# Gate products inside attention, and slots inverted to tokens so that experts gather rows of x

## The chip, the cores and the metric

The kernel runs on one core of a Trainium2 chip. The metric is the device time in microseconds of one launch, which covers all stages. Inputs and output are float32 arrays in HBM.

## What is computed

```python
# attention: B, H, S, D = 4, 8, 768, 40; for every step t of S
y[:, :, t] = einsum('bhd,bhde->bhe', rt, state)
Sa = einsum('bhde,bhe->bhd', state, at)
state = state * wt - outer(Sa, bt) + outer(vt, kt)
x = y.transpose(0, 2, 1, 3).reshape(3072, 320)
# routed experts: E = 8, F = 1024
noisy = x @ w_gate + log1p(exp(x @ w_noise)) * noise
top2, top2_w = the two largest of the 8 and their softmax
out[token] = sum over its two experts e of top2_w * (relu(x[token] @ w1[e]) @ w2[e])
# feed-forward: h = out @ w_in (320 x 2048), g = h * tanh(softplus(h)), result g @ w_out
```

## The kernel before

`build` runs four stages one after another: `attention`, `route`, `experts`, `mish_ffn`. Each is a `Block` in which every engine has its own instruction list; at its end all engines meet at a barrier.

**attention** works on 8 groups of 4 heads (GR = 8), 12 chunks of 64 steps each. One TensorE list is written out by the string `ORDER`: single letters `u`, `s`, `r` are the hops of the recurrence, short and each waiting for the one before; the tokens with a digit (`N0`, `K1`, `F0`, `X1`) are wide steps of 6 to 48 matmuls into one of three PSUM buffers `wide`, which are placed between the hops. ScalarE (`BY_ACT`) or VectorE takes each buffer away. `Y` makes the output transposed in `yT`; `X` (L431 to L436) turns `yT` back into rows of tokens, six transposes a step, and ScalarE copies them to `xr` (L511 to L516). There are 16 X steps, two per group. SP stores `xr` to `x_by_pair` in HBM. Near the start ScalarE's queue also writes zeros to all of `slots` (L522).

**route** reads x back (L719) into `xg`, tokens on partitions, 24 tiles of 128. TensorE transposes each tile (L758), ScalarE and VectorE copy it (L774, L799), and TensorE multiplies it by the gate weights into `plog` (L746). Then VectorE makes the noisy logits, the two best experts, ranks within each expert (two matmuls, L766 and L767) and `pos`, the slot of each token's two choices (L803 to L852). Slots are sorted by expert, padded to 55 tiles of 128 (M = 55). GpSimd scatters the rows of `xg` to `slots` by 48 indirect DMAs (L739), each of which follows the last one, and waits until they have landed. `tile_expert` (L857) tells which expert each tile belongs to. SP loads the down weights of all experts after the noise (L721 and L1223).

**experts** runs over the 55 tiles: SP loads a tile of `slots` into `xs` (L903) and that expert's up weights (L909, L911), TensorE transposes x (L932), multiplies up (L943, L948) and down (L962). VectorE copies the result and GpSimd's queue stores it to `results` (L922). TensorE's list is hidden(t), turn_x(t+1), output(t-1).

**mish_ffn** gathers each token's two result rows by indirect DMAs on `pos` (L1073), mixes them and runs the feed-forward.

## Time and profile before

| what | us |
|---|---|
| median of 3 runs (lowest, highest) | 1735.26 (1734.24, 1742.23) |
| the profiled execution | 1734.15 |
| its span | 1732.4 |
| attention, until the barrier behind it | 595.4 |
| route, until the experts' first transfer | 138.2 |
| experts, until the last stage's first transfer | 539.5 |
| TensorE busy in the span | 1458.0 (84%) |
| VectorE, ScalarE, GpSimd busy | 582.3, 580.1, 285.8 |

The stage bounds are the first instructions behind each barrier at 595.40, 733.64 and 1273.17 us. A time of the profile counts from the start of the span. The granted clock of TensorE is 0.5 where it is at 1.2 GHz and 1.0 where it is at 2.4 GHz. Lines named L... are those of the kernel before.

### The profile page before, as it was taken

Reading aid. Unit: us, or ns where it says so; the run is one execution under the profiler, and the core shown is the slowest. Engines: PE = TensorE matmul, PEld = TensorE weight load, DVE = VectorE, ACT = ScalarE, POOL = GpSimd, SP = SyncE. Lnnn points to the kernel's source line nnn. Section 1 sums busy time; section 2 is a strip of 40 time slices with the busy share of each in tenths; the row PEclk is TensorE's granted clock in tenths of the full one; section 3 lists DMA queues with packets and bytes.
Section 4 is the critical chain, followed back from the end, with each engine's and each line's share of the span. In section 5 each row is a group of like instructions: output and inputs, shape, how many; then the busy total and the mean of one; then the engine's idle time right before and its main releaser. Section 6 shows DMA issues by size and latency. Waiting matters only on the chain. (4 is left out here: it accounts for less than half of the span.)

```text
span 1732.4 us, 42914 instructions
## 1 busy us (share of the span) xinstructions
PE 1458.0 (84%) x18753; PEld 1126.9 (65%) x18753; DVE 582.3 (34%) x1120; ACT 580.1 (33%) x1145; POOL 285.8 (16%) x253
## 2 busy tenths in 40 slices
PE   1687887888897590089999999999948999999999
PEld 1577776777786490078888888888823555555556
DVE  8454664564543113000000000000016545445441
ACT  0353554454453110011121211212108454555541
POOL 5333223223210004600000000000041101000000
PEclk9878998888887655589999999999969999999999
DMA  7524134224111292375656555565361101000000
GB/s 213 154 52 111 45 76 117 66 54 117 47 46 42 56 298 76 111 241 162 186 163 184 174 169 186 159 188 166 105 185 35 31 23 31 27 23 12 8 12 19
DMA packets 127671, 180.66 MB, mean 104 GB/s; under 512 B 68384, under 2 KB 96800, under 8 KB 126208
## 3 DMA queue, kind: packets, MB, share of 16 engines
q1 hardware_dynamic: 113184, 144.16, 29.1%
q0 software_dynamic: 7248, 24.75, 4.3%
q10 hardware_dynamic: 7056, 9.01, 1.5%
q8 instruction: 151, 2.47, 0.6%
q14 instruction: 32, 0.26, 0.1%
HBM read 144.13 MB, written 33.75 MB: 103 GB/s over the span
## 5 line engine op out<-in xcount | busy, mean ns | idle before, releaser
L962 PE MATMUL pY<-down,hT 128*128 x880 | 245.9, 433 | 0.0
L998 DVE COPY ys<-pY 128x320 f32<-128x320 f32 x55 | 27.0, 491 | 570.9 <-PE pY L962 570.9
L943 PEld LDWEIGHTS pH<-exT,up 128*128 128x128 f32 x1760 | 207.7, 194 | 14.5 <-DMA up_rest<-in_moe_w 4.4
L943 PE MATMUL pH<-exT,up 128*128 128x128 f32 x1760 | 208.3, 277 | 5.4 <-DMA up_rest<-in_moe_w 3.9
L1108 PE MATMUL mpY<-wout,h 128*128 128x320 f32 x768 | 210.4, 433 | 0.0
L962 PEld LDWEIGHTS pY<-down,hT 128*128 128x128 f32 x880 | 163.0, 190 | 61.2
L989 ACT ACTIVATE hT<-pH 128x512 f32<-128x512 f32 x110 | 59.7, 594 | 422.1 <-PE pH L948 422.1
L1108 PEld LDWEIGHTS mpY<-wout,h 128*128 128x128 f32 x768 | 144.3, 190 | 60.7 <-issue 3.0
L1095 PE MATMUL mpH<-mxT,win 128*128 128x512 f32 x384 | 173.2, 605 | 4.9 <-ACT mxT L1137 4.7
L1095 PEld LDWEIGHTS mpH<-mxT,win 128*128 128x128 f32 x384 | 74.0, 194 | 92.1 <-issue 82.7
L1145 ACT ACTIVATE act_in<-act_in 128x512 f32<-128x512 f32 x96 | 59.9, 629 | 183.2 <-DVE act_in L1184 183.2
L922 POOL DMA_DIRECT2D results<-ys x55 | 29.8, 541 | 509.5 <-DVE ys L998 509.5
L1175 DVE TENSOR_TENSOR h<-h,act_in 128x512 f32<-128x512 f32 x96 | 59.9, 685 | 142.8 <-ACT act_in L1151 142.7
L932 PE MATMUL pX<-ident,xs 128*128 128x128 f32 x110 | 24.4, 304 | 75.4 <-DMA xs<-slots 75.4
L1184 DVE TENSOR_SCALAR act_in<-mpH 128x512 f32<-128x512 f32 x96 | 65.4, 682 | 59.4 <-PE mpH L1098 59.4
L1073 POOL DMA_INDIRECT rows<-results,pos x48 | 45.7, 953 | 230.8 <-DVE mix L1163 214.7
L484 ACT ACTIVATE npow<-wide 128x768 bf16<-128x768 f32 x80 | 63.3, 810 | 55.8 <-PE wide L373 37.9
L484 ACT ACTIVATE uv<-chain 64x80 f32<-64x80 f32 x192 | 44.1, 230 | 93.8 <-PE chain L456 92.3
L282 POOL TENSOR_TENSOR kbT<-kbT,after 128x1536 f32<-128x1536 f32 x16 | 55.0, 3457 | 107.6 <-DMA kbT<-in_kb 107.6
L411 PE MATMUL wide<-rblk,uvT 80*128 80x128 f32 x384 | 61.4, 324 | 6.7 <-issue 5.7
L1185 DVE COPY h<-mpH 128x512 f32<-128x512 f32 x96 | 65.1, 678 | 0.0
L932 PEld LDWEIGHTS pX<-ident,xs 128*128 128x128 f32 x110 | 11.2, 142 | 82.4 <-DMA xs<-slots 75.9
(168 smaller groups left out, 2167.7 us busy)
## 6 DMA issues: line engine op xcount, KB each, us to landing
up<-in_moe_w SPq DMA_DIRECT2D x55, 1024.0 KB, 5.3
up_rest<-in_moe_w SPq DMA_DIRECT2D x110, 128.0 KB, 5.3
down<-in_moe_w SPq DMA_DIRECT2D x8, 1280.0 KB, 14.7
slots<-zero_row ACTq DMA_DIRECT2D x1, 8800.0 KB, 36.2
xs<-slots SPq DMA_DIRECT2D x55, 160.0 KB, 5.2
results<-ys POOLq DMA_DIRECT2D x55, 160.0 KB, 2.2
wfr<-in_wdec SPq DMA_DIRECT2D x16, 480.0 KB
kbT<-in_kb SPq DMA_DIRECT2D x16, 480.0 KB
```

Source lines behind the costliest of these rows:

```text
L282: nc.gpsimd.tensor_tensor(kbT[:, i], kbT[:, i], backwards, ALU.mult).then_inc(kb_scaled, 1)
L411: m = pe.matmul(out[:, bank, place], uvT[half][:, i, c].rearrange("q s f -> q (s f)"), rblk[half][:, i, c].rearrange("q h f -> q (h f)"), ...
L484: return nc.scalar.activation(out, in_, ACT.Copy, scale=scale)
L943: pe.matmul(pH[t % 2][b][:, c, :], up[t % NU][:, k, f * P:(f + 1) * P], xT[t % 2][:, k, :], start=(c == 0 and k == 0), stop=False, skip_gr ...
L962: m = pe.matmul(pY[t % 2][:, 0:D], hT[t % 2][:, j, :], down[:, bass.ds(e, 1), j, :].rearrange("q n d -> q (n d)"), start=(j == 0), stop=(j ...
L989: nc.scalar.activation(hT[t % 2][:, b * HT:(b + 1) * HT, :], pH[t % 2][b][:], ACT.Relu).then_inc(h_copied[b], 1)
L1095: pe.matmul(pH[f % 4][:], win[:, k, f * P:(f + 1) * P], xT[g % 2][:, k, :], start=(k == 0), stop=False)
L1108: m = pe.matmul(pY[t % 2][:, 0:D], h[g % 2][:, f, j * P:(j + 1) * P], wout[:, f, :], start=(f == 0), stop=(f == FT - 1))
L1145: nc.scalar.activation(a[:, f, :], a[:, f, :], ACT.Exp).then_inc(exped, 1)
L1175: nc.vector.tensor_tensor(at, at, act_in[n % 3][:, f, :], ALU.mult).then_inc(gated, 1)
L1184: nc.vector.tensor_scalar(act_in[n % 3][:, f, :], pH[f][:], 20.0, None, ALU.min).then_inc(h_min, 1)
L1185: nc.vector.tensor_copy(h[g % 2][:, GT * q + f, :], pH[f][:]).then_inc(h_used, 1)
```

## The change

The routing stage no longer touches x. In attention the X step multiplies `yT`, which has the features on the partitions, by the gate weights of the group's heads (`gw`, loaded once) into 48 free columns of the same PSUM buffer. Two groups make up one batch element's features: the second one adds the sum so far, which is in `logits`, by a matmul with the identity. ScalarE copies the 48 columns to `logits`.

In `route`, after `pos` is known as a float, each slot is split into its tile (of 55) and its row (of 128). For each of the 48 pairs of token tile and choice, VectorE makes `row_hot` (a token's row as 0/1 over 128) and, over the 55 tiles, the token's tile number where it matches; GpSimd makes the same with the row of the token. TensorE multiplies and sums over all 48, so that `slot_token` holds for each slot the number of its token. In `experts`, GpSimd gathers the rows of x by indirect DMAs on `slot_token`. The scatter to `slots`, `slots` itself and its zeros are gone. The noise transfer is the first of its stage on SP's queue and the down weights follow.

```diff
+                    if g == 0:
+                        pe.wait_ge(gate_loaded, 16)
+                    else:
+                        taken(pe, tok, g - 1)
+                    first, odd = g // 2 * (S // P) + half * (W // P), g % 2 == 1
+                    if odd:
+                        pe.matmul(out[:, 0, W:W + W // P * 2 * E], ident[:], logits[:, first:first + W // P, :].rearrange("q c n -> q (c n)"),
+                                  start=True, stop=False, skip_group_check=True)
+                    for j in range(W // P):
+                        for i in range(2):
+                            m = pe.matmul(out[:, 0, W + j * 2 * E:W + (j + 1) * 2 * E], yT[:, i, cols(j, P)], gw[:, g % 2 * 2 + i, :],
+                                          start=(i == 0 and not odd), stop=(i == 1), skip_group_check=True)
...
+                        copy(xr[:, i, rows, :].rearrange("q c (h d) -> q c h d", d=D),
+                             t[:, i, 0:W].rearrange("q (c h d) -> q c h d", h=2, d=64)[:, :, :, 0:D])
+                    first = g // 2 * (S // P) + half * (W // P)
+                    m = copy(logits[:, first:first + W // P, :], t[:, 0, W:W + W // P * 2 * E].rearrange("q (c n) -> q c n", n=2 * E))
...
-            act.wait_ge(kb_loaded, 32)
-            act.dma_start(slots.rearrange("(m q) d -> q m d", q=P),
-                          zero_row[:].unsqueeze(1).to_broadcast([P, slots.shape[0] // P, slots.shape[1]])).then_inc(slots_cleared, 16)
...
-            for b in range(B):
-                for j in range(4):
-                    sp.dma_start(xg[:, b * NC:(b + 1) * NC, j * 80:(j + 1) * 80],
-                                 x_by_pair[4 * b + j].rearrange("(c q) d -> q c d", q=P)).then_inc(rows[b], 16)
-            sp.dma_start(nz[:], noise.rearrange("(t q) e -> q t e", q=P)).then_inc(wload, 16)
+            sp.dma_start(nz[:], noise.rearrange("(t q) e -> q t e", q=P)).then_inc(nload, 16)
...
-            pool.wait_ge(placed, 1)
-            for t in range(T):
-                for k in range(2):
-                    nc.gpsimd.indirect_dma_start(out=slots, out_offset=bass.IndirectOffsetOnAxis(ap=pos[:, 2 * t + k:2 * t + k + 1], axis=0),
-                                                 in_=xg[:, t, :], in_offset=None).then_inc(sent, 16)
-            pool.wait_ge(sent, 32 * T)
...
+            pool.wait_ge(split_up, 1)
+            for j in range(2 * T):
+                nc.gpsimd.tensor_scalar(tile_hot[:, j, 1, :], minus_m[:], minus_tile[:, j // 2, j % 2:j % 2 + 1], row_of[:],
+                                        ALU.is_equal, ALU.mult).then_inc(by_pool, 1)
...
+            for j in range(2 * T):
+                pe.wait_ge(by_dve, j + 1)
+                pe.wait_ge(by_pool, j + 1)
+                m = pe.matmul(pinv[:], row_hot[:, j, :], tile_hot[:, j], start=(j == 0), stop=(j == 2 * T - 1))
+            m.then_inc(inverted, 1)
...
+            then(vec.tensor_scalar(tile_i[:], posf[:], 1.0 / P, None, ALU.mult))
+            then(vec.tensor_copy(tile_f[:], tile_i[:]))
+            then(vec.scalar_tensor_tensor(row[:], tile_f[:], -float(P), posf[:], ALU.mult, ALU.add))
+            then(vec.scalar_tensor_tensor(minus_tile[:], row[:], 0.0, tile_f[:], ALU.is_lt, ALU.subtract))
+            vec.scalar_tensor_tensor(row[:], minus_tile[:], float(P), posf[:], ALU.mult, ALU.add).then_inc(split_up, 1)
+            dve.wait_ge(split_up, 1)
+            for j in range(2 * T):
+                vec.tensor_scalar(tile_hot[:, j, 0, :], minus_m[:], minus_tile[:, j // 2, j % 2:j % 2 + 1], float(j // 2), ALU.is_equal, ALU.mult)
+                vec.tensor_scalar(row_hot[:, j, :], iota_row[:], row[:, j // 2, j % 2:j % 2 + 1], None, ALU.is_equal).then_inc(by_dve, 1)
+            then(vec.tensor_copy(pos[:].rearrange("q (t k) -> q t k", k=2), posf[:]))
...
+            dve.wait_ge(inverted, 1)
+            then(vec.tensor_copy(texp[:], pinv[:, 1, :]))
+            then(vec.scalar_tensor_tensor(slot_token[:], pinv[:, 0, :], float(P), texp[:], ALU.mult, ALU.add))
...
-            def load_x(t):
-
-                wait(sp, x_turned, t - 2)
-                sp.dma_start(xs[t % 3][:], xv[t]).then_inc(loaded[t % 3], 16)
...
+            def gather_x(t):
+
+                wait(pool, x_turned, t - 2)
+                nc.gpsimd.indirect_dma_start(out=xs[t % 3][:], out_offset=None, in_=x,
+                                             in_offset=bass.IndirectOffsetOnAxis(ap=slot_token[:, t:t + 1], axis=0)).then_inc(loaded[t % 3], 16)
+
+            for t in range(3):
+                gather_x(t)
             for t in range(M):
+                if t + 3 < M:
+                    gather_x(t + 3)
```

TensorE's list around X0 in attention, of a second group (g = 1) before, and now. `wide` is the PSUM buffer; the rows ahead and behind are F0 and F1 and the chain's last hop.

```order
L387 MATMUL wide<-tpow,npow 64x64 x23
L435 MATMUL wide<-ident,yT 128x128 [waits wide_taken_by_dve]
L435 MATMUL wide<-ident,yT 128x128 x5
L387 MATMUL wide<-tpow,npow 64x64 [waits wide_taken_by_dve,wide_taken_by_act]
L387 MATMUL wide<-tpow,npow 64x64 x23
L456 MATMUL chain<-rhs,w 64x40 [waits rhs_ready]
```

```order
L389 MATMUL wide<-tpow,npow 64x64 x23
L437 MATMUL wide<-ident,yT 128x128 [waits wide_taken_by_dve]
L437 MATMUL wide<-ident,yT 128x128 x5
L445 MATMUL wide<-logits,ident 128x48 [waits wide_taken_by_act]
L449 MATMUL wide<-gw,yT 128x16 x6
L389 MATMUL wide<-tpow,npow 64x64 [waits wide_taken_by_dve,wide_taken_by_act]
L389 MATMUL wide<-tpow,npow 64x64 x23
L471 MATMUL chain<-rhs,w 64x40 [waits rhs_ready]
```

Seven matmuls now stand between the transposes and F1. The end of VectorE's list in the routing stage, from the sum that gives the slot as a float (`posf`), before and now (two of the 48 pairs are shown):

```order
L850 TENSOR_REDUCE posf<-chosen 128x24
L852 CAST pos<-posf 128x2x24 [waits gate_steps]
L854 TENSOR_TENSOR past<-iota_m,last 128x440
L856 TENSOR_REDUCE texp<-past 128x55 [waits gate_steps]
L857 TENSOR_SCALAR tile_expert<-texp 128x55 [waits gate_steps]
```

```order
L823 TENSOR_REDUCE posf<-chosen 128x24
L827 TENSOR_SCALAR tile_i<-posf 128x48 [waits gate_steps]
L828 CAST tile_f<-tile_i 128x48 [waits gate_steps]
L829 SCALAR_TENSOR_TENSOR row<-tile_f,posf 128x48 [waits gate_steps]
L830 SCALAR_TENSOR_TENSOR minus_tile<-row,tile_f 128x48 [waits gate_steps]
L831 SCALAR_TENSOR_TENSOR row<-minus_tile,posf 128x48 [waits gate_steps]
L834 TENSOR_SCALAR tile_hot<-minus_m,minus_tile 128x55 [waits slots_split]
L835 TENSOR_SCALAR row_hot<-iota_row,row 128x128
L834 TENSOR_SCALAR tile_hot<-minus_m,minus_tile 128x55
L835 TENSOR_SCALAR row_hot<-iota_row,row 128x128
```

`pos` and `tile_expert` now come behind the 48 pairs. GpSimd's queue from the end of the routing stage into the experts, before and now:

```order
L733 AFFINE_SELECT before<-before 128x128 [waits gate_constants]
L739 DMA slots<-xg,pos 7040x320 [waits slots_known]
L739 DMA slots<-xg,pos 7040x320 x47
L663 UNCONDITIONAL_BRANCH [waits rows_sent]
L918 UNCONDITIONAL_BRANCH [waits barrier_Pool_Activation_PE_DVE_SP_gather]
L922 DMA results<-ys 128x320 [waits y_copied] x55
```

```order
L740 TENSOR_SCALAR tile_hot<-minus_m,minus_tile,row_of 128x55 [waits slots_split,gate_constants]
L740 TENSOR_SCALAR tile_hot<-minus_m,minus_tile,row_of 128x55 x47
L673 UNCONDITIONAL_BRANCH
L897 UNCONDITIONAL_BRANCH [waits barrier_Pool_Activation_PE_DVE_SP_gather]
L902 DMA xs<-x,slot_token 128x320 x3
L902 DMA xs<-x,slot_token 128x320 [waits x_turned]
L911 DMA results<-ys 128x320 [waits y_copied]
L902 DMA xs<-x,slot_token 128x320 [waits x_turned]
L911 DMA results<-ys 128x320 [waits y_copied]
```

The 48 scatters are gone from the routing stage, and a gather stands ahead of each store but the last three in the experts' stage.

## Rows read from the trace of the kernel before

**Rows 1.** Stages, by stretch: length, busy of PE, PEld, DVE, ACT, POOL, clock, DMA.
```profile
607.00:649.00 42.00, 41.63 (x207) 41.10 (x205) 7.12 (x23) 5.82 (x22) 0.00 (x0) 0.50 1.03 303
667.00:733.00 66.00, 0.00 (x0) 0.00 (x0) 0.90 (x2) 0.00 (x0) 46.09 (x48) 0.50 0.33 119
751.00:1271.00 520.00, 514.33 (x3631) 431.28 (x3630) 27.01 (x55) 95.08 (x267) 29.75 (x55) 1.00 0.53 165
```
**Rows 2.** Timeline (start, duration, engine, instruction), around the barrier behind attention.
```profile
591.81 0.63 ACT L484 ACTIVATE xr<-wide 128x240 f32<-128x240 f32 x2 [7.79 <-PE wide L435]
595.40 0.14 POOL L727 IOTA iota_e<- 128x8 f32 x1 [97.54 <-POOLq L94]
```
**Rows 3.** Timeline, VectorE's routing chain.
```profile
648.67 0.36 DVE L803 TENSOR_SCALAR relz<-plog 128x192 f32<-128x192 f32 x1 [4.32 <-PE plog L746]
...
651.52 0.36 DVE L807 TENSOR_TENSOR relz<-relz,lnz 128x192 f32<-128x192 f32 x1 [2.10 <-ACT lnz L780]
...
666.17 0.19 DVE L852 CAST pos<-posf 128x48 int32<-128x48 f32 x1
```
**Rows 4.** Timeline, start of the experts.
```profile
733.64 0.34 SPq L903 DMA_DIRECT2D xs<-slots  x1
...
741.17 4.21 PE L943 MATMUL pH<-exT,up 128*128 128x128 f32 x18 [3.91 <-DMA up_rest<-in_moe_w]
```
**Rows 5.** DMA: noise (L721) from issue to landing, and the down weights' issues.
```profile
DMA to landing us min/median/max: 4.9/4.9/4.9
```
```profile
down<-in_moe_w SPq DMA_DIRECT2D x8, 1280.0 KB, 14.7
```
**Rows 6.** VectorE prices: two operations with a pointer scalar (min/median/max ns), and a cast's timeline.
```profile
L1159 DVE TENSOR_SCALAR mix<-rows,gates x24: 376/379/407, 1282.2 to 1611.1; 128x320 f32<-128x320 f32 x24
L1161 DVE SCALAR_TENSOR_TENSOR mix<-rows,gates,mix x24: 550/550/602, 1282.7 to 1611.5; 128x320 f32<-128x320 f32 x24
```
```profile
22.83 0.20 DVE L626 CAST identh<-ident 128x128 bf16<-128x128 f32 x1
22.94 0.18 DVE L630 COPY eye<-ident 64x64 f32<-64x64 f32 x1
```
**Rows 7.** Timeline, VectorE beside GpSimd.
```profile
31.81 2.69 POOL L287 MEMSET aT<- 128x1536 f32 x2
```
```profile
31.84 2.74 DVE L630 CAST eyeh<-ident 64x64 bf16<-64x64 f32 x1
```
```profile
667.56 0.38 DVE L857 TENSOR_SCALAR tile_expert<-texp 128x55 int32<-128x55 f32 x1
```
**Rows 8.** Timeline, GpSimd's own operations.
```profile
5.95 0.28 POOL L268 TENSOR_SCALAR_AFFINE_SELECT n<-n 128x128 f32<-128x128 f32 x1
...
22.99 1.80 POOL L275 TENSOR_TENSOR aT<-aT,dec 128x768 f32<-128x768 f32 x1 [2.17 <-DVE dec L597]
```
**Rows 9.** Timeline, TensorE prices: a wide f32 product, and weight loads in the experts.
```profile
659.36 0.98 PE L766 MATMUL pbef<-both,before 128*128 128x192 f32 x2 [10.73 <-DVE both L824]
```
```profile
760.02 3.81 PEld L943 LDWEIGHTS pH<-exT,up 128*128 128x128 f32 x32
```
**Rows 10.** Stretches ahead of the barriers behind the routing and behind attention, columns as in rows 1.
```profile
729.00:729.50 0.50, 0.00 (x0) 0.00 (x0) 0.00 (x0) 0.00 (x0) 0.00 (x0) 0.50 0.00 0
```
```profile
594.50:595.00 0.50, 0.00 (x0) 0.00 (x0) 0.00 (x0) 0.00 (x0) 0.00 (x0) 0.50 0.00 0
```
**Rows 11.** Indirect reads of rows (L1073) to landing; a result's store and tile 4's first transpose.
```profile
DMA to landing us min/median/max: 2.9/3.3/7.5
```
```profile
761.29 0.59 POOL L922 DMA_DIRECT2D results<-ys  x1 [33.89 <-DVE ys L998]
...
774.50 0.44 PE L932 MATMUL pX<-ident,xs 128*128 128x128 f32 x2
```
**Rows 12.** Steady attention, columns as in rows 1; TensorE's waits for the scaled keys: us, times, longest.
```profile
120.00:480.00 360.00, 301.51 (x9272) 268.14 (x9271) 202.51 (x363) 170.04 (x429) 103.88 (x54) 0.87 0.32 78
```
```profile
PE wide L336 <- POOL kbT L282: 7.7, 3, 5.1
```

More of the change, by code:

```diff
@@ L69, in attention @@
     HOPS = 3 * NC - 2
+    E = gate_w.shape[2] // 2
     def group_of(tok, it):
@@ L210, in store @@
                 rows = slice(half * (HC // 2), (half + 1) * (HC // 2))
+                first, pair = g // 2 * S + half * W, g % 2 * 2
                 for i in range(2):
-                    sp.dma_start(out_v[2 * g + i][:, rows, :], xr[:, i, rows, :]).then_inc(x_stored[half], 16)
+                    sp.dma_start(x[first:first + W, (pair + i) * DD:(pair + i + 1) * DD].rearrange("(c q) d -> q c d", q=P),
+                                 xr[:, i, rows, :]).then_inc(x_stored[half], 16)
             sp.wait_ge(w_pads, 1)
@@ L652, in _, with route @@
                         take(tok, g)
-def route(nc, x_by_pair, w_gate, w_noise, noise, slots, pos, gates, tile_expert, ident, load_down):
+def route(nc, logits, noise, pos, gates, tile_expert, slot_token, ident, load_down):
     N, E = noise.shape
-    D = w_gate.shape[0]
     T = N // P
-    B = x_by_pair.shape[0] // 4
-    NC = T // B
     M = tile_expert.shape[1]
@@ L752, in _ @@
-            for t in range(T):
-                if t % NC == 0:
-                    pe.wait_ge(rows[t // NC], 64)
-                wait(pe, copied[t % 2], t // 2 - 1)
-                for k, (k0, kn) in enumerate(KT):
-                    m = pe.transpose(pT[t % 4][0:kn, k, :], xg[:, t, k0:k0 + kn], ident[:])
-                m.then_inc(turned, 1)
-                if t > 2:
-                    logit(pe, t - 3)
-            for t in range(T - 3, T):
-                logit(pe, t)
             pe.wait_ge(const, 2)
@@ L769, in _ @@
+            m.then_inc(inverted, 1)
         @block.scalar
         def _(act):
-            for t in range(0, T, 2):
-                act.wait_ge(turned, t + 1)
-                wait(act, logits, t - 3)
-                nc.scalar.activation(xT[t % 4][:, 0, :], pT[t % 4][:, 0, :], ACT.Copy)
-                nc.scalar.activation(xT[t % 4][0:96, 1:3, :], pT[t % 4][0:96, 1:3, :], ACT.Copy).then_inc(copied[0], 1)
             act.wait_ge(soft, 1)
```

113 lines of the change are left out of this document (47 added, 66 removed).

## Prediction

> **What bounds the kernel now.** I read the stage table first. In the expert stage TensorE works 514.33 of 520 us and in 607 to 649 us 41.63 of 42, but from 667 to 733 us neither TensorE, VectorE nor ScalarE does anything and only GpSimd works [rows 1]. So four stages run one after another (attention, routing, experts, feed-forward), each shut off by a barrier, and what a stage costs is its own longest path. The routing stage is where the change acts. Its path starts with the barrier after attention, 595.40 us [rows 2]. The rows of x are read back, and then TensorE is the path until the last gate product; VectorE starts at 648.67 [rows 3]. That stretch is 53.3 us. VectorE then ranks the tokens until it writes pos at 666.17: 17.5 us [rows 3]. GpSimd issues 48 scatters one by one; the next stage's first transfer is issued at 733.64 and its first matmul starts at 741.17 [rows 4]. From 595.40 to 741.17 is 145.8 us, of which the change keeps little.
>
> **Removed in routing.** All 72 transposes, 144 gate matmuls, their copies, the 16 reads of x and the 48 scatters go. VectorE can start at the barrier: minus 53.3 us. The scatters and what follows them, 666.17 to 733.64, go too: minus 67.5 us; what stands in their place is costed below. The 9 MB of zeros that were written to slots during attention's first microseconds go as well. I count nothing for them, since no wait in the sum is on that queue.
>
> **The VectorE chain that stays** is 17.5 us. In it the noise is used at 651.52, which is 2.85 us after the chain's start [rows 3]. The noise transfer is now the first thing of its stage and landed 4.9 us after its issue [rows 5], so VectorE waits about 2.3 us for it (0 if it lands within 2.85 us, 5 if the down weights queued right behind on SP's queue slow it). Five small operations on 128x48 that split a slot into tile and row follow; at the 0.19 us of the pos cast [rows 3] and a semaphore wait each, 0.24 us, that is 1.2 us.
>
> **The inversion** is new: for each of 48 columns VectorE makes one 128x55 and one 128x128 comparison in bf16, GpSimd one 128x55, TensorE one matmul. The nearest VectorE row is a comparison's sister with a pointer scalar: 379 ns for 320 elements [rows 6]. Its two-tensor neighbour of the same length takes 550 ns [rows 6]: 171 ns more for 320 elements, 0.53 ns each, which I read as the one-source form costing 0.53 ns an element. So 128 elements cost 379 - 192 x 0.53 = 0.28 us and 55 cost 0.24 us. The next instruction starts about 0.09 us before the former ends (22.83 plus 0.20 against 22.94 [rows 6]). So a pair costs 0.19 + 0.15 = 0.34 us and 48 pairs 16.3 us. If the pointer cost nothing it would be some 10 us.
>
> GpSimd works at the same time and takes part in that price. In this trace a 64x64 cast that started at 31.84 lasted 2.74 us, until the two memsets of GpSimd were done, and a 128x55 operation lasted 0.38 us, ending when a GpSimd descriptor instruction ended [rows 7]. So short VectorE operations with one source in SBUF stand still while GpSimd holds something. A GpSimd select over 128 elements lasts 0.28 us [rows 8]; for 55 elements I take 0.2. If each of the 48 blocks VectorE for its whole length, the inversion is 48 x (0.34 + 0.2) = 26 us; if only the data parts exclude one another it adds about half, 21 us. I take 21, since the fixed part of a short instruction is most of it, and keep 10 and 26.
>
> The Trainium skill, "SBUF — State Buffer", section "Who interferes with whom", says that a VectorE instruction in a 2-port mode and a GpSimd instruction take a shared port pair for the whole instruction, whichever comes first, and the other fully blocks. By that rule the inversion would be the 26 us and the time 1657. The 2.74 us row agrees with it; no row shows two short instructions alternating.
>
> TensorE's matmul per column is hidden: a 128x192 f32 product, two records, took 0.98 us at the low clock [rows 9]; 110 bf16 columns in one record cost at most a third of that, 0.33 us, less than a pair. After the last column VectorE does pos, past, texp and tile_expert, as before from 666.17 to 667.94, 1.77 us [rows 3, 7], and two more short ones: 2.3 us.
>
> Sum from the barrier: 17.5 + 2.3 + 1.2 + 21 + 2.3 = 44.3 us.
>
> **The next barrier.** Before, the DMA engines were idle from 729.0 on, yet the experts' first transfer came at 733.64, 4.6 us later; after attention they were idle from 594.5 and GpSimd began at 595.40, 0.9 us later [rows 2, 4, 10]. The difference is that GpSimd had transfers outstanding in one case. In the changed routing stage it has none, so I take 0.4 us (bounds 0.2 and 4.6).
>
> **First rows of the experts.** The first expert matmul came 7.5 us after the stage's first transfer, because of the up weights [rows 4]. SP is now free of the x loads, so the weights come a little earlier, but x is fetched by GpSimd with an indirect read: one issue of 1.0 us, a landing of 2.9 to 7.5 us by the like reads of the last stage [rows 11], then transposes and copies. I take 8.0 us, bounds 7.2 and 10.5. The down weights are the stage's next transfers, 8 of 1280 KB [rows 5], 10.5 MB; at the 303 GB/s of [rows 1] they take 35 us and are in at 632, before anyone asks.
>
> First expert matmul: 595.4 + 44.3 + 0.4 + 8.0 = 648.1 instead of 741.2, **minus 93.1 us**.
>
> **Steady experts.** POOL now holds a gather ahead of each store. The gather of tile t+3 stands behind the store of tile t-1, which waits for VectorE's copy. For t = 1 that store is issued at 761.29 and tile 4 is turned at 774.50 [rows 11]: 13.2 us less 0.6 and 1.0 for the issues and a landing of 3.3 (7.5 at worst) leaves 8 us (4). The gather is hidden and the stage keeps its length. If that cover were gone, each microsecond would count 55 times.
>
> **Added in attention.** Each of 16 X steps gets six matmuls with 128x128 f32 weights, and every second group one matmul of the identity over 48 columns. Such matmuls are bound by their weights: 32 loads in 3.81 us, 0.119 each [rows 9]. That is 16 x 6 x 0.119 = 11.4 us, and 8 more for the four odd groups, 1.0 us: 12.4 us of TensorE. From 120 to 480 us TensorE works 301.5 of 360 us [rows 12], in program order with the chain's short hops between, so I count most of it. What can hide it: TensorE waited three times, 7.7 us in all, for GpSimd's scaled keys behind X0 [rows 12], which does not move with X0; that takes 2.4 us off. I take 10 us on the path, bounds 4 and 15 (the extra may delay the hops, and ScalarE's third copy in X, below the 0.32 us of one of its two [rows 2], sits ahead of a hop's copy). At the end of attention that copy adds 0.2 us.
>
> **Total**: 1734.15 (the profiled execution; the span is 1732.4, 1.75 less) - 93.1 + 10.2 = 1651.3. The median of the three runs is 1.1 us above the profiled one, so I say 1652.
>
> **Rivals.**
> - *GpSimd sets the inversion*: a comparison with two pointers and two operations takes 0.5 us there instead of 0.2 and is excluded with VectorE's: 48 x 0.84 = 40 us, 1671. For it: GpSimd's two-input products cost 1.80 us for 768 elements, more than twice a VectorE element [rows 8]. Against: 55 elements at that rate are 0.13 us.
> - *Everything overlaps*: X hidden down to 4 us and no port trouble, 16.3 or 10 us: 1652 - 6 - 5 to -11 = 1635 to 1641. For it: one sixth of TensorE's time in attention is idle. Against: the only wait in it that I can name beside X is the 7.7 us taken off already.
> - *Attention pays twice*: the X step delays a hop as well as the wide steps behind it, 24 us instead of 10: 1666. For it: hops wait for each other in one chain. Against: TensorE works 301.5 of 360 us there, which leaves the hops little to hold up [rows 12].
> - *Slower than before*: the gathers gate the experts, since GpSimd takes its queue in order behind the store's wait. It needs landings of 8 us more than I took, plus 83/55 = 1.5 us per tile to eat the gain, about 13 us each; from there the time is above 1735. The worst like landing was 7.5 us [rows 11].
> - *The change does not shorten the stage as it says*: the down weights, now issued at once, become its end. At half the rate of [rows 1] they would land at 667 and the experts' weights behind them: 1679.
>
> **How the numbers follow.** Forecast (1640 to 1662) 64%, GpSimd-bound 11%, all overlapped 11%, attention twice 8%, down weights 3%, gathers slower than before 2%, near no change by several at once 1%. The range 1634 to 1672 takes in the first four and the unknowns' bounds, and leaves 6 to 15%. A measurement of this kernel tells 0.5% (8.7 us) from nothing; faster by more 0.97, within 0.01, slower 0.02.
>
> **What would show it.** VectorE's first routing operation right at the barrier; a wait of some 2 us before the noise is used; 48 pairs of comparisons spaced 0.34 (no contention) to 0.54 us (full exclusion); under 1 us from the last VectorE operation to the experts' first transfer; L943's first matmul some 8 us behind; expert tiles still 9.45 us apart; attention's end near 605 instead of 595. I would be wrong if a comparison costs over 0.5 us on either engine, or if the hops slip by more than TensorE's extra work.

## The result

The kernel after takes 1693.7 us (median of 4 runs, 1681.85 to 1701.33) against 1735.67 us before, a ratio of 0.974 with a 95% interval of 0.969 to 0.980. It is faster by 2.6%. The prediction said 1652 us, 1634 to 1672: the direction was right, the size was not, and the time lies 22 us above the range.

The profiled execution took 1690.76 us (span 1689.0), where the sum of the prediction was 1651.3. These 39.5 us can be placed stage by stage, as each stage is shut off from the next by a barrier:

| piece of the path | predicted | measured | error |
|---|---|---|---|
| attention's end, later than before by | 10.2 | 37.9 (595.40 to 633.31) | +27.7 |
| barrier to the first comparison | 21.0 | 19.35 (to 652.66) | -1.65 |
| inversion | 21 | 30.9 (to 683.58) | +9.9 |
| what follows the inversion | 2.3 | 0.5 (to 684.05) | -1.8 |
| barrier to the experts | 0.4 | 1.25 (to 685.30) | +0.85 |
| first fetch to first expert matmul | 8.0 | 8.05 (to 693.35) | 0 |
| first expert matmul to last copy, change | 0 | 523.1 instead of 524.2 | -1.1 |
| last copy of the experts to the next stage, change | 0 | 12.3 instead of 7.8 | +4.5 |
| feed-forward, change | 0 | 460.2 instead of 459.2 | +1.0 |

Two terms carry the error: attention and the inversion. A third, the barrier behind the experts, wasn't in the sum at all. What follows the inversion took 0.5 us and not 2.3, since VectorE made `pos`, `past`, `texp` and `tile_expert` by 671.5 us, while GpSimd was still at its comparisons.

### The profile page after: what moved, and what is told of

It is laid out like the page before. It is cut to its first block and busy times, and to the rows that moved or that the text cites. A ratio compares the mean times of both kernels' runs of the same rounds, so it can differ in the third digit from the quotient of the medians.

```text
span 1689.0 us, 43070 instructions
## 1 busy us (share of the span) xinstructions
PE 1474.6 (87%) x18793; PEld 1138.5 (67%) x18793; DVE 597.6 (35%) x1198; ACT 575.3 (34%) x1137; POOL 326.6 (19%) x311
## 5 line engine op out<-in xcount | busy, mean ns | idle before, releaser
L413 PE MATMUL wide<-rblk,uvT 80*128 80x128 f32 x384 | 72.2, 365 | 1.0 <-ACT uvT L499 1.0
L413 PEld LDWEIGHTS wide<-rblk,uvT 80*128 80x128 f32 x384 | 66.6, 270 | 2.5 <-ACT uvT L499 1.2
L338 PE MATMUL wide<-kbT,aT 40*64 40x64 f32 x768 | 23.4, 291 | 50.9 <-DVE mask_un L648 38.6
L471 PE MATMUL chain<-rhs,w 64*64 64x40 f32 x768 | 48.4, 247 | 20.1 <-issue 7.6
```

The lines of the kernel that those rows point to most:

```text
L413: m = pe.matmul(out[:, bank, place], uvT[half][:, i, c].rearrange("q s f -> q (s f)"), rblk[half][:, i, c].rearrange("q h f -> q (h f)"), ...
```

## The profile after

**Attention.** The timeline of the kernel after, around attention's end, answers to [rows 2] (start, duration, engine, instruction, and in brackets the idle time before it and what ended it):

```profile
612.09 0.63 ACT L499 ACTIVATE xr<-wide 128x240 f32<-128x240 f32 x2 [7.19 <-PE wide L449]
...
629.23 0.63 ACT L499 ACTIVATE xr<-wide 128x240 f32<-128x240 f32 x2 [13.41 <-PE wide L449]
629.75 0.22 ACT L499 ACTIVATE logits<-wide 128x48 f32<-128x48 f32 x1
```
```profile
633.31 0.14 POOL L726 IOTA iota_e<- 128x8 f32 x1 [109.82 <-POOLq L95]
```

The last X step and the barrier behind it come 37.9 us later than in [rows 2]. Next, the X step's own price: one step's gate products on TensorE's timeline, first at the full clock, then near the end, where the granted clock is 1.00 up to 611 us and 0.50 from 612 on, and the groups of matmuls by line and shape (busy us, mean ns of one, idle before):

```profile
138.91 1.41 PE L449 MATMUL wide<-gw,yT 128*128 128x16 f32 x12
```
```profile
610.23 1.82 PE L449 MATMUL wide<-gw,yT 128*128 128x16 f32 x12
```
```profile
L449 PE MATMUL wide<-gw,yT 128*128 128x16 f32 x192 | 25.1, 270 | 0.0
L437 PE MATMUL wide<-ident,yT 128*128 128x128 f32 x96 | 16.0, 310 | 4.8 <-DVE yT L593 4.3 <-ACT npow L499 0.2
L445 PE MATMUL wide<-logits,ident 128*128 128x48 f32 x16 | 2.7, 251 | 0.0
```

Six f32 matmuls leave twelve records, while the six transposes of a step leave six (96 for 16 steps). A step's products cost 12 x 0.117 = 1.41 us, not 0.71. (The records of a group overlap: one lasts 270 ns in the mean, yet 192 of them make 25.1 us.) All in all the new records are 25.1 + 2.7 = 27.8 us of busy time. The last view is attention as one stretch from its start to its end, of before and of after (length, busy of PE, PEld, DVE, ACT, POOL with counts, granted clock, DMA share, GB/s):

```profile
0.00:595.00 595.00, 451.95 (x13432) 400.11 (x13432) 319.89 (x548) 250.04 (x625) 162.93 (x96) 0.86 0.33 84
```
```profile
0.00:633.00 633.00, 500.74 (x13640) 450.82 (x13640) 324.20 (x547) 251.67 (x641) 163.37 (x96) 0.82 0.27 65
```

TensorE has 208 records more and is busy 48.8 us more. 27.8 of these are the new records; the other 21 are the same old instructions taking longer, and the granted clock fell from 0.86 to 0.82. Between 1.2 GHz (0.5) and 2.4 GHz (1.0), a mean clock c says that the engine was at the lower level for 2(1 - c) of the time: 167 us before, 228 us after (to some 6 us, since c has two digits).

**Routing.** The timeline of the inversion in the kernel after, first VectorE's comparisons, then GpSimd's (joined into one line of 48), TensorE's last products, and the experts' first fetch:

```profile
652.42 0.21 DVE L831 SCALAR_TENSOR_TENSOR row<-minus_tile,posf 128x48 f32<-128x48 f32 x1
652.66 0.25 DVE L834 TENSOR_SCALAR tile_hot<-minus_m,minus_tile 128x55 bf16<-128x55 f32 x1
652.83 0.28 DVE L835 TENSOR_SCALAR row_hot<-iota_row,row 128x128 bf16<-128x128 f32 x1
653.02 0.24 DVE L834 TENSOR_SCALAR tile_hot<-minus_m,minus_tile 128x55 bf16<-128x55 f32 x1
```
```profile
652.81 30.26 POOL L740 TENSOR_SCALAR tile_hot<-minus_m,minus_tile,row_of 128x55 bf16<-128x55 f32 x48 [17.77 <-DVE row L831]
685.30 1.19 POOL L902 DMA_INDIRECT xs<-x,slot_token  x1 [2.23 <-POOLq L673]
```
```profile
682.67 0.25 PE L752 MATMUL pinv<-tile_hot,row_hot 128*128 128x110 bf16 x1 [0.29 <-POOL tile_hot L740]
683.22 0.25 PE L752 MATMUL pinv<-tile_hot,row_hot 128*128 128x110 bf16 x1 [0.30 <-POOL tile_hot L740]
```

A pair of VectorE's comes every 0.36 us and the last ends at 669.87 us. GpSimd is then still at it for 13 us, and TensorE waits for it each time. The tile's own view (min/median/max ns) has the price of each:

```profile
L834 DVE TENSOR_SCALAR tile_hot<-minus_m,minus_tile x48: 237/242/310, 652.7 to 669.4; 128x55 bf16<-128x55 f32 x48
L740 POOL TENSOR_SCALAR tile_hot<-minus_m,minus_tile,row_of x48: 564/646/965, 652.8 to 682.5; 128x55 bf16<-128x55 f32 x48
```

**Experts.** The first expert matmul, the landings of the gathers, and the last copy with the next stage's first transfer, 12.3 us apart:

```profile
693.35 5.33 PE L932 MATMUL pH<-exT,up 128*128 128x128 f32 x32 [1.00 <-DMA up_rest<-in_moe_w]
```
```profile
DMA to landing us min/median/max: 2.9/2.9/6.8
```
```profile
1216.49 0.49 DVE L987 COPY ys<-pY 128x320 f32<-128x320 f32 x1 [3.81 <-PE pY L951]
```
```profile
1228.82 0.84 SPq L1042 DMA_DIRECT2D win<-in_moe_w_in  x2
```

The same two rows of the kernel before, 7.8 us apart:

```profile
1265.37 0.49 DVE L998 COPY ys<-pY 128x320 f32<-128x320 f32 x1 [3.81 <-PE pY L962]
```
```profile
1273.17 0.84 SPq L1053 DMA_DIRECT2D win<-in_moe_w_in  x2
```

## Experiments on attention: records or clock

Two questions stood open: is it the products at all, and if so, their own time or the clock that went with them? The runs in this section are compared by their times and by attention's end, read as the start of GpSimd's first instruction behind the barrier. An end is that of one execution, the profiled one. From it to the end of the span it took 1054.1 to 1057.4 us in the nine profiled executions whose later stages are those of the kernel after (the fused one adds a single VectorE addition), so the ends of the other executions can be estimated as their span less 1056: 624 to 644 for the kernel after, 589 to 612 without products, 603 to 612 with 128 columns.

The end moves with the clock even where the program is the same. The kernel after, its repetition, and the two runs below in which ScalarE makes the second comparison or issues the stores have the same attention with 13640 records in it. They ended it at 633.31, 633.35, 640.30 and 651.83 us, with TensorE busy for 500.7, 500.6, 509.2 and 517.4 us and a granted clock of 0.82, 0.81, 0.80 and 0.79. The last of them:

```profile
0.00:651.00 651.00, 517.43 (x13640) 464.69 (x13640) 324.51 (x547) 251.63 (x641) 163.95 (x96) 0.79 0.27 63
```

**Without the products.** In the X step all six gate matmuls, the addition of the former group and the copy of the logits go, so that the noise alone routes:

```
-                        for j ...: for i ...: m = pe.matmul(out[:, 0, W + ...], yT[:, i, ...], gw[...], ...)
-                    m = copy(logits[:, first:first + W // P, :], ...)
+                            m = pe.transpose(out[:, i, cols(j, P)], yT[:, i, cols(j, P)], ident[:])
```

> Leaves out the gate products: attention makes no logits (they stay zero and the noise alone routes), everything else is the kernel after. Theory A (the 208 new matmul records are the cause, by their own time, 27.8 us, and by the lower granted clock that goes with them, some 21 us on the others, less idle time that closed): attention's last copy ends near 595 us, as before, against 633 after, the window of attention has TensorE busy 452 us at a clock of 0.86 instead of 501 us at 0.82, and the whole is 38 us shorter, 1652 us. Rival B (the attention of the kernel after is long for another reason, the transfers of gate weights, the wait for the logits' copy or a clock that happened to be low in that execution): the end stays above 615 us.

Measured: 1662.4 us (1646.6 to 1669.7), ratio 0.955 (0.947 to 0.963), attention's end at 605.29 us. The products, with the copy that goes with them, are the cause: 31 us come back. The end isn't at 595, though: this execution had a clock of 0.85 and so 182 us of low clock instead of 167.

**Half of them.**

```
-                        for i in range(2):
-                            m = pe.matmul(..., yT[:, i, cols(j, P)], gw[:, g % 2 * 2 + i, :], ...)
+                        m = pe.matmul(..., yT[:, 0, cols(j, P)], gw[:, g % 2 * 2, :], ...)
```

> Leaves out every second gate product (the upper half of each group's rows of the gate weights), 96 of the 192 product records; routing differs. Theory A with a cost in proportion to the records: attention's end half way, near 614 us, time 1672 us. Rival C (the cost comes in a step, because the step exists at all, with its waits and the copy of the logits): the end is within 5 us of 633 us, time about 1690 us.

Measured: 1664.9 us (1657.9 to 1671.5), ratio 0.957 (0.952 to 0.962), end at 612.98 us with a clock of 0.83. The profiled execution, the slowest of the four at 1671.5 us, came where the first expectation had put it (614 and 1672), but the median is 7 us below, and only 2.5 us above the run without products. Leaving out half of the records brings nearly the whole gain: by the medians the cost isn't in proportion to their number.

**The same products, 128 columns.**

```
-    m = pe.matmul(out[:, 0, W + j * 2 * E:...], yT[:, i, cols(j, P)], gw[:, g % 2 * 2 + i, :], ...)
+    m = pe.matmul(out[:, 0, W:W + P], yT[:, i, cols(j, P)], ident[:], start=True, stop=True, ...)
```

> The same number of products with the same stationary operand, but 128 moving columns of the identity instead of 16 of the gate weights: the logits are meaningless, routing differs. If a product costs its weight load and a fixed part, whatever its columns (theory A), the step takes what it takes in the kernel after, 1.4 us for 12 records at the full clock, and attention ends at 633 us or, should more columns keep the granted clock up, some us earlier. If columns set the price (rival D), it ends 10 us or more later, as the 12 records take 0.117 us each now and 96 transposes of 128 columns stand beside them at their own rows' price.

Measured: 1667.9 us (1660.4 to 1669.6), ratio 0.960 (0.956 to 0.965), end at 604.23 us, 29 us before that of the kernel after, with as many records. I had thought of a few us at best. Against the run without products, on the same chip, the 208 records cost 5.5 us in the median, with ranges that overlap. That isn't their price at an equal clock, which was 0.88 here and 0.85 there; no run isolates it. Part of it fell into time in which TensorE had stood idle: 150.5 us of attention without products, 134.6 here.

**The kernel after again, and with the gate weights padded** with zeros to 96 columns, which computes what the kernel after does:

```
-        gw = sb("gw", [P, 4, gate_w.shape[2]])
+        gw = sb("gw", [P, 4, 96])                                # columns 16 to 95 are zero
-    m = pe.matmul(out[:, 0, W + j * 2 * E:W + (j + 1) * 2 * E], yT[...], gw[...], ...)
+    m = pe.matmul(out[:, 0, W + j * 2 * E:W + j * 2 * E + 96], yT[...], gw[...], ...)
```

> The kernel after, once more, on the chip on which the next three run, since the end of attention lay between 633 and 652 us in the kernels so far that leave attention as the change made it. Expected: end of attention 630 to 652 us, 1685 to 1700 us.

> The kernel after with the gate weights padded with zeros from 16 to 96 moving columns; nothing is left out and no record is added or taken away. Theory N (what makes attention long is the granted clock, and it falls because the products have few columns; they cost their 0.12 us each whatever their width): attention ends near 605 us, as with 128 columns of the identity, against 633 to 652, and the whole is 25 us shorter, near 1668 us. Rival O (the gain with 128 columns came from the other routing that it brought, or from that chip): no gain, 1690 us.

Measured on one chip: 1698.1 us (1691.8 to 1700.4), ratio 0.976 (0.969 to 0.983), for the kernel after again, with attention's end at 633.35; 1679.2 us (1662.9 to 1683.7), ratio 0.966 (0.958 to 0.973), padded. Every padded run is below every one of the other. The padded end is 606.63 us in the profiled execution, which was the fastest of its four; the others' are 618 to 626 by the estimate above. The gain is 19 us in the median, where 25 had been expected; the 128 columns stood 26 us below the kernel after, on another chip. To make room one mask is stored once and read six times over; VectorE's busy time doesn't show it (318.46 us below, against 319.85), and the run with 128 columns has its gain without that edit. Their stretches of attention, the kernel after again, then padded, then those with 128 columns and without products, columns as above:

```profile
0.00:633.00 633.00, 500.55 (x13640) 449.86 (x13640) 319.85 (x547) 251.54 (x641) 162.57 (x96) 0.81 0.27 65
```
```profile
0.00:606.00 606.00, 469.43 (x13640) 420.08 (x13640) 318.46 (x547) 251.72 (x641) 162.83 (x97) 0.88 0.28 68
```
```profile
0.00:604.00 604.00, 469.41 (x13640) 419.42 (x13640) 319.09 (x547) 251.15 (x641) 162.65 (x96) 0.88 0.29 68
```
```profile
0.00:605.00 605.00, 454.54 (x13432) 402.69 (x13432) 321.12 (x547) 249.78 (x625) 162.88 (x97) 0.85 0.29 68
```

The first three have 13640 matmul records each. With 16 columns TensorE needs 31 us more for them, while it stands idle no longer (132.5 us against 136.6 and 134.6), and the clock is 0.81 instead of 0.88: 241 us at 1.2 GHz instead of 145. A wide product costs hardly more than a narrow one. Padded, one step at the full clock and the group of all products read

```profile
134.91 1.48 PE L451 MATMUL wide<-gw,yT 128*128 128x96 f32 x12
```
```profile
L451 PE MATMUL wide<-gw,yT 128*128 128x96 f32 x192 | 25.4, 285 | 0.0
```

against 1.41 and 25.1 us for 16 columns. Little of the time is lost in the X steps themselves: 13 of the 16 steps of the kernel after ran their products at a clock of 0.90 or above. It is lost behind them. In the stretch of 480 to 540 us the kernel after had 0.79, which is 25 us at the lower level, and the padded one 1.00 (the two are not at quite the same place of the program there):

```profile
480.00:540.00 60.00, 52.45 (x1523) 47.44 (x1517) 23.63 (x49) 27.56 (x69) 15.26 (x8) 0.79 0.24 61
```
```profile
480.00:540.00 60.00, 53.68 (x1725) 48.08 (x1725) 29.85 (x60) 31.61 (x81) 10.32 (x7) 1.00 0.18 45
```

Where the clock falls can be read in stretches of 1 us from the start of each step's products (in the kernels without products or with the fused ones, of its transposes). In the kernel after and in its repetition it went from 1.00 to 0.50 within 4 us of that start in 8 of 16 steps each, with the stores from ScalarE's queue and with the zeros in 10 of 16; with half of the products in 3; padded, with 128 columns and fused in none; in the kernel before and without products in one, the last. The eleventh step, whose products start at 495.18 us in the kernel after and at 481.13 us in the padded one, shows both, with the stretch of the step and the five us behind it:

```profile
495.00:498.00 3.00, 2.31 (x50) 2.19 (x51) 0.96 (x1) 1.07 (x5) 0.26 (x1) 0.98 0.02 5
499.00:504.00 5.00, 5.00 (x135) 4.32 (x138) 1.23 (x3) 1.87 (x5) 0.82 (x1) 0.50 0.65 163
```
```profile
481.00:484.00 3.00, 2.31 (x51) 2.12 (x49) 0.95 (x1) 1.07 (x5) 0.90 (x1) 1.00 0.03 5
485.00:490.00 5.00, 4.59 (x188) 4.10 (x187) 3.07 (x5) 2.33 (x7) 1.08 (x2) 1.00 0.65 153
```

TensorE was as busy in the two steps (2.31 of 3.00 us). So narrow products brought the lower clock, and wide ones in their place took it away again; behind which of the steps it falls can't be told in advance from these runs.

**Another order.** Each gate product stands behind the transpose of the same piece:

```
+                            pe.transpose(out[:, i, cols(j, P)], yT[:, i, cols(j, P)], ident[:])
                             m = pe.matmul(out[:, 0, W + ...], yT[:, i, cols(j, P)], gw[...], ...)
```

> The same matmuls as in the kernel after, but each gate product stands directly behind the transpose of the same piece, so that the narrow ones are no longer twelve records in a row; nothing is left out. Theory P (a row of narrow matmuls brings the granted clock down): attention ends near 605 us, 1668 us. Rival Q (their number counts, not their order): 633 to 652 us, 1690 us.

Measured: 1687.7 us (1674.5 to 1693.3), ratio 0.968 (0.960 to 0.976), end at 629.94 us with a clock of 0.81. That is 10 us below the kernel after on the same chip, with intervals that overlap, and nowhere near 605. That the narrow records stand in a row isn't the cause. In this kernel a transpose starts between two parts of a sum in the same PSUM bank, and the logits come out as other numbers, so it routes otherwise. "PSUM — Partial Sum Buffer" of the Trainium skill, section "The four PSUM rules", says that the first matmul of a sum clears the written bits over its whole zero region; that would explain it, but no run here tests it.

**Turning and products in one matmul.** The identity's 80 needed columns and the 16 gate columns lie side by side; VectorE adds the partial products. For room the three masks are stored once, not six times:

```
-    pe.transpose(out[:, i, cols(j, P)], yT[:, i, cols(j, P)], ident[:])      # six, then the six products
+    m = pe.matmul(out[:, i, cols(j, DD + 2 * E)], yT[:, i, cols(j, P)], turner[:, g % 2 * 2 + i, :], start=True, stop=True, ...)
```

> Nothing is left out: the identity and the gate weights lie side by side in one moving operand of 96 columns, so that one matmul of each piece of the transposed rows gives both the turned rows and the gate products (the two halves and the two groups are added by VectorE). The 16 x 6 products and the 8 additions are gone as matmuls of their own: TensorE has 208 records less. Theory A: attention ends within 8 us of the kernel before, 595 to 603 us, time 1655 to 1662 us. Rival B (something other than these records makes attention long): above 615 us. Rival E (a two-pass matmul of 96 columns costs far more than a transpose): L445's step grows from 0.7 to over 1.5 us and the gain is below 15 us.

Measured: 1670.0 us (1663.7 to 1678.7), ratio 0.963 (0.956 to 0.969), end at 609.02 us, clock 0.84 in attention. That lies between the two expectations of 603 and 615 us. Against the kernel before, attention has 96 records more, not none, since six matmuls leave twelve records where six transposes left six (13528 against 13432). The step takes 1.55 us for its twelve records of 96 columns:

```profile
134.56 1.55 PE L446 MATMUL wide<-turner,yT 128*128 128x96 f32 x12 [0.52 <-DVE yT L589]
```

Some 24 us of the 31 come back, with nothing left out.

**The zeros.** The writing of 9 MB of zeros is put back, in pieces half as long as in the kernel before:

```
+            act.dma_start(slots..., zero_row[:]...to_broadcast(...)).then_inc(slots_cleared, 16)
```

> The kernel after with the zeroing of 9 MB put back into attention, from ScalarE's queue (in pieces of 640 bytes instead of 1280, for want of room). If taking it out brought time in attention (theory J: TensorE had 118 more records done in the 38 to 60 us window, about 4 us), the kernel is 3 to 5 us longer. If the lead is used up by waits later on (rival K): within 1 us.

Measured: 1704.9 us (1693.6 to 1708.0), ratio 0.978 (0.974 to 0.983), end at 652.21 us. Its times overlap with both sets of the kernel after, and on the same chip the run with the stores from ScalarE, below, ended attention at 651.83 us without zeros. Whether the zeros cost anything can't be told; it's no large part of either sum.

## Experiments on the inversion and the barrier

**ScalarE makes the second comparison** as a scaled copy of VectorE's first:

```
-                nc.gpsimd.tensor_scalar(tile_hot[:, j, 1, :], minus_m[:], minus_tile[...], row_of[:], ALU.is_equal, ALU.mult)
+                act.wait_ge(by_dve0, j + 1)
+                nc.scalar.activation(tile_hot[:, j, 1, :], tile_hot[:, j, 0, :], ACT.Copy, scale=scale[:, j // 2:j // 2 + 1])
```

> The second comparison of the inversion, on GpSimd in the kernel after, is replaced by a ScalarE copy of VectorE's first one, scaled by a number of each row; the result is the same. Theory F (GpSimd sets the inversion: 48 comparisons, 30.3 us, against VectorE's 48 pairs, 17.1 us): the stretch from VectorE's split to the reading of the slots' tokens falls from 31 to 18 us, the bound is VectorE's pairs again, 13 us less, 1677 us. Rival G (TensorE's products or their waits bound it, as they follow the comparisons closely): less than 4 us.

Measured: 1682.1 us (1680.7 to 1684.3), ratio 0.967 (0.964 to 0.971). Attention ended at 640.30 us in the profiled execution, so the comparison is best made behind it: the first fetch comes 39.7 us after the barrier instead of 52.0. That is 12.3 us less, where 13 had been expected; the 1677 us were missed by 5, and attention ended 7 us later here than in the kernel after. The tile's views show both engines now in step:

```profile
L839 DVE TENSOR_SCALAR tile_hot<-minus_m,minus_tile x48: 246/249/253, 659.6 to 676.2; 128x55 bf16<-128x55 f32 x48
L765 ACT ACTIVATE tile_hot<-tile_hot,scale x48: 339/340/342, 659.9 to 676.5; 128x55 bf16<-128x55 bf16 x48
```

VectorE's own pace is the same as beside GpSimd: its first comparison is repeated 47 times in 16.6 us, 0.353 us each, against (669.4 - 652.7)/47 = 0.355 us in the kernel after. So GpSimd did not hold VectorE up. It was the other way round, if anything: GpSimd's first 21 comparisons took 0.69 us each while VectorE worked; at the end, with VectorE done, they came every 0.55 us (the products that wait for them, 682.67 and 683.22 us above). Why, no run shows.

```profile
652.81 14.54 POOL L740 TENSOR_SCALAR tile_hot<-minus_m,minus_tile,row_of 128x55 bf16<-128x55 f32 x21 [17.77 <-DVE row L831]
```

**What GpSimd asks for a comparison.**

> Adds twenty comparisons on scratch behind GpSimd's last one in routing, four of each: 55 elements with two numbers per row (the form of the change), 128 elements of the same, 55 with one number per row, 55 with one constant, 55 with two constants. Theory L (my 0.2 us came from an operation with constants, and the two numbers per row are what costs): 0.58 us for the first, below 0.3 us with constants. Rival M (any GpSimd operation of this length takes 0.5 us or more): all within 0.1 us of each other at 55 elements, and 128 elements take longer by the length alone.

Measured, four of each, on GpSimd's timeline (one execution, 1706.2 us):

```profile
690.57 2.20 POOL L744 TENSOR_SCALAR probe<-minus_m,minus_tile,row_of 128x55 f32<-128x55 f32 x4
692.75 3.14 POOL L746 TENSOR_SCALAR probe<-iota_row,minus_tile,row_of 128x128 f32<-128x128 f32 x4
695.88 1.61 POOL L748 TENSOR_SCALAR probe<-minus_m,minus_tile 128x55 f32<-128x55 f32 x4
697.46 1.27 POOL L750 TENSOR_SCALAR probe<-minus_m 128x55 f32<-128x55 f32 x4
698.80 1.87 POOL L752 TENSOR_SCALAR probe<-minus_m 128x55 f32<-128x55 f32 x4
```

Per operation: 0.55 us with two numbers per row, 0.40 with one, 0.32 with one constant, 0.47 with two constants; 73 elements more add 0.24 us, 3.2 ns each. The first form had been expected at 0.58, the one constant below 0.3: neither theory is right as stated. The length is a third of the price (55 x 3.2 ns = 0.18 us), the second operation costs about 0.15, numbers per row instead of constants 0.08, be it one or two. The plainest form is above the 0.2 us of the prediction, too.

**Stores from ScalarE's queue.**

```
-                pool.wait_ge(y_copied, t + 1)
-                pool.dma_start(yv[t], ys[t % 2][:]).then_inc(stored[t % 2], 16)
+                act.wait_ge(y_copied, t + 1)
+                act.dma_start(yv[t], ys[t % 2][:]).then_inc(stored[t % 2], 16)
```

> The experts' 55 result stores are issued from ScalarE's queue instead of GpSimd's; nothing is left out. GpSimd has 55 DMAs in the stage instead of 110, as the scatters were 48 before. Theory H (the stage's closing wait grows with the DMAs that GpSimd issued in it, some 0.09 us each: 4.6 us at 48, 9.9 us at 110): 11.5 us between the last store and the next stage's first transfer fall to about 7, 5 us less in all, 1686 us. Rival I (the wait is for something else, such as the completion of the last gather or store): unchanged at 11 to 12 us.

Measured: 1695.7 us (1683.8 to 1703.9), ratio 0.974 (0.968 to 0.980). The total shows nothing, as attention ended at 651.83 us in the profiled execution; but the way from the last copy to the next stage does. It took 12.31 to 12.33 us in each of the eleven profiled executions in which GpSimd issues both the gathers and the stores. Here it reads:

```profile
1234.93 0.49 DVE L993 COPY ys<-pY 128x320 f32<-128x320 f32 x1 [3.82 <-PE pY L947]
```
```profile
1237.64 0.84 SPq L1048 DMA_DIRECT2D win<-in_moe_w_in  x2
```

2.7 us instead of 12.3. It fell by 9.6 us where I had said 5. So it hangs on what GpSimd issues, but 0.09 us for each one in the stage isn't the law. With 55 gathers still issued there, the price is nearly gone. The last gather is now long past when the stage ends; whether that is the reason, or whether only stores count, wasn't tried.

**All three.** The fused matmul, ScalarE's comparison, and the stores from ScalarE's queue:

> Three edits in one, nothing left out: products and turning in one matmul of 96 columns, the second comparison of the inversion by ScalarE, the experts' stores issued from ScalarE's queue. By the single runs: attention ends near 607 us, attention's end to the first fetch 40 us instead of 52 (inversion 17 instead of 30), the last copy of the experts to the next stage 2.7 us instead of 12.3. Sum from the 1670 us of the first edit alone: less 12, less 9.6, 1648 us. Should the edits get into each other's way (the second comparison and the additions on VectorE, the stores in front of ScalarE's copies), above 1655 us.

Measured: 1643.5 us (1639.2 to 1650.4) against 1741.5 us of the kernel before on that chip, ratio 0.945 (0.938 to 0.952), and 55 us less than the kernel after on the same chip. The barrier to the first fetch takes 40.0 us and the last copy to the next stage 2.7:

```profile
603.59 0.14 POOL L733 IOTA iota_e<- 128x8 f32 x1 [104.36 <-POOLq L95]
```
```profile
643.56 1.19 POOL L914 DMA_INDIRECT xs<-x,slot_token  x1 [38.08 <-POOLq L677]
```

The three gains add up: 1670.0 - 12.3 - 9.6 = 1648 us, and the run is 5 us below that. It is the best of all the kernels here, with the reference's computation left whole.

## Why the prediction was wrong, point by point

- **"Each of 16 X steps gets six matmuls ... 0.119 each"** failed, in its price. That came from [rows 9], where 32 weight loads take 3.81 us. Those were records, and an f32 matmul leaves two of them, as the first row of [rows 9] has it ("a 128x192 f32 product, two records", the prediction says itself). The step was 1.41 us and not 0.71, and TensorE's extra work 27.8 us and not 12.4. Whether the 10 us taken for the path would have been right at an unchanged clock isn't shown; the nearest comparison, 128 columns against none, gives 5.5 us in the median at a somewhat better clock. The routing stage of the kernel before had the very product, with 16 moving columns, three matmuls as six records (the "144 gate matmuls" that go are 72, too):

```profile
607.23 1.30 PE L746 MATMUL plog<-wgn,gxT 128*128 128x16 f32 x6
```

- **The clock wasn't a term of the sum: this step failed most.** "I take 10 us on the path, bounds 4 and 15" holds only if attention keeps its clock, 0.87 in [rows 12]. It fell from 0.86 to 0.82 over the whole of attention, and the old matmuls lengthened with it. The medians put this at some 19 us (padded against after, same chip) to 26 (128 columns against after, different chips). With the double count it put attention's end at 633 instead of 605. A sign had stood in [rows 1]: from 607 to 649 us, where TensorE does nothing but those products and transposes, it is busy for 41.63 of 42 us and has a granted clock of 0.50. The figure of the rival "attention pays twice" (24 us instead of 10) was nearer, but its mechanism, late hops, isn't what the runs show. TensorE's waits for the hops' copies were alike in both kernels, as the waits of the kernel after show (waiting line, releaser: us in total, times, longest): before they were 9.0 us for ScalarE's and 6.5 for VectorE's.

```profile
PE chain L478 <- ACT uv L499: 8.9, 26, 0.8
...
PE chain L471 <- DVE rhs L617: 6.9, 19, 1.0
```

- **"for 55 elements I take 0.2"** failed. GpSimd's comparison took 0.55 us alone and 0.69 beside VectorE. I had scaled a GpSimd instruction of another kind ([rows 8]) down by its length. The rival "GpSimd sets the inversion" was the right one of the two: its own price of 0.5 us was near, its 40 us were too much, as it also added VectorE's pairs on top, which run beside. The prediction had named this sign of being wrong itself, "a comparison costs over 0.5 us on either engine".
- **"short VectorE operations with one source in SBUF stand still while GpSimd holds something"** failed for these operations: 0.355 us a pair beside GpSimd, 0.353 without it. The 2.74 us in [rows 7] was no rule for them. Had each engine stood still for the whole of the other's instruction, GpSimd's 0.55 us would have made it 48 x (0.34 + 0.55) = 43 us, and the 48 comparisons took 30.3. The exclusive rule of "SBUF — State Buffer" in the Trainium skill, "Who interferes with whom", is set beside it in the prediction; the same section says that a VectorE instruction with at most one SBUF input outside the 2-port modes doesn't contend. VectorE's pace agrees with the latter, GpSimd's 0.69 against 0.55 us doesn't, and in which mode these comparisons ran no run shows.
- **The pair itself, 0.34 us**, was right (0.355), and so were the noise's wait (2.83 us against 2.3), the split (1.2 us both) and that TensorE's products are hidden by the comparisons.
- **The barriers.** Behind the routing 1.25 us instead of 0.4, within the bounds. Behind the experts I had no term: with a gather beside each store, it grew from 7.8 to 12.3 us. The prediction read in [rows 10] that a barrier came 4.6 us after the last transfer where GpSimd had some outstanding and 0.9 us after it elsewhere, and asked this of the routing stage only.
- **Held:** first fetch to first expert matmul 8.05 us (8.0); the gathers hidden, landing in 2.9 to 6.8 us; the experts' stage as long as before within 1.1 us; the down weights no bound.

Of the range, its upper end of 1672 took the GpSimd rival or the attention rival, one at a time. Both terms were too small at once, and the barrier behind the experts was missing. The direction was right for the reason given: the routing stage's path, from attention's end to the first expert matmul, fell from 145.8 to 60.0 us.

## What to carry to other kernels

Count TensorE's work in the records that the profile counts: an f32 matmul is two, a transpose one. Where a tuned stage runs at a mixed granted clock, give the clock a term of its own when narrow matmuls are added, and try them padded, or joined to a wide matmul of the same stationary operand. Price a GpSimd operation only from the same form, and look what GpSimd has still issued when a stage closes: moving its stores to another queue took 9.6 us from the way into the next stage.

## What had not been expected of the hardware

- Twelve records of 16 moving columns, each with a fresh f32 weight load, took 1.41 us at the full clock and twelve of 96 columns 1.48, yet the kernel with the wide ones ran 19 us faster in the median, with attention's granted clock at 0.88 instead of 0.81 in the profiled executions.
- The clock fell mostly behind those steps, not in them: within 4 us of the products' start in 8 of 16 steps with 16 columns, in none with 96 or 128.
- The granted clock of attention wanders between executions of one program. The spans of the unchanged kernel after reach from 1680.1 to 1699.6 us, while in nine profiled executions with the same later stages all that follows attention took 1054.1 to 1057.4 us, and the routing stage 51.8 to 52.1; a part's effect is better read between two barriers than from the total.
- From the last copy of the experts' stage to the next stage's first transfer it took 7.8 us where GpSimd issued 55 stores, 12.3 us with 55 stores and 55 gathers, and 2.7 us where it had only gathers, long done.
- GpSimd's comparison costs 0.32 us for 55 elements even with one constant and 0.55 with two numbers per row; ScalarE's scaled copy of the same 55 elements took 0.34 us and kept VectorE's pace.
